# Attention scores in one plain fp32 product instead of two products on split operands

## The reference, cut to what matters

```
q_bucket = sum((q @ proj > 0) * 2**bit)          # k_bucket likewise
mask     = q_bucket[:, None] == k_bucket[None, :]
scores   = where(mask, scale * q @ k.T, -1e9)
attn     = softmax(scores)                       # over the keys
out      = attn @ v                              # fp32
```

## Time and profile before

| | |
|---|---|
| median of 3 runs | 672.47 us (672.25 to 673.8) |
| span of the profiled execution | 672.3 us |
| its mean granted TensorE clock | 0.990 |
| PE busy, of the span | 638.7 us, 95% |
| DVE, ACT, POOL busy | 54%, 46%, 37% |

### The profile page before, as it was taken

How to read it: one execution, slowest core, us unless ns; L and a number is a source line. 1 busy time by engine, 2 the same in 40 slices (tenths; PEclk the granted TensorE clock), 3 DMA queues, 4 the chain that set the end, 5 groups by cost and what they waited for, 6 DMA issues and landing times.

```text
span 672.3 us, 11293 instructions
## 1 busy us (share of the span) xinstructions
PE 638.7 (95%) x3810; PEld 512.0 (76%) x3810; DVE 364.8 (54%) x599; ACT 307.5 (46%) x586; POOL 250.7 (37%) x202
## 2 busy tenths in 40 slices
PE   2899999999999999888999999999999999996998
PEld 1667576766666675888888888889888888885786
DVE  3878786968778785987211111116333333369720
ACT  2877776868686773355322222223222222251132
POOL 6543333334252341844333333326444444342130
PEclk9999999999999999989999999999999999998899
DMA  5822231324132000100222221520222221000102
GB/s 125 248 71 71 71 94 47 94 68 112 56 91 71 0 25 1 48 1 0 64 63 62 62 62 62 188 63 30 65 62 62 62 62 47 1 0 1 62 32 94
DMA packets 34262, 42.08 MB, mean 63 GB/s; under 512 B 3520, under 2 KB 22208, under 8 KB 34240
## 3 DMA queue, kind: packets, MB, share of 16 engines
q1 hardware_dynamic: 32512, 37.77, 19.6%
q0 software_dynamic: 1728, 4.02, 2.3%
HBM read 38.63 MB, written 3.15 MB: 62 GB/s over the span
## 4 chain that ended last, share of the span: by engine, by line
PE 81%; DVE 11%; issue 3%; POOL 2%; ACT 1%; DMA 1%; SPq 0%; DVEq 0%; POOLq 0%; ACTq 0%
PE banks L1457 20%; PE banks L1445 20%; PE banks L1260 10%; PE banks L1243 10%; PE banks L1307 6%; PE banks L1552 5%; DVE row_min L927 2%; PE banks L1199 2%; PE banks L1536 2%; DVE x_then_u_then_gate L1135 2%; PE banks L1380 2%; PE banks L1432 1%; DVE x_then_u_then_gate L1132 1%; DVE probT L342 1%; DVE k_b L920 1%
## 5 line engine op out<-in xcount | busy, mean ns | idle before, releaser
L1122 DVE SCALAR_TENSOR_TENSOR h_lo<-banks,h_hi 128x512 fp32r<-128x512 f32 x64 | 35.5, 558 | 180.8 <-ACT h_hi L825 180.8
L927 DVE TENSOR_REDUCE row_min<-banks 128x1 f32<-128x768 f32 x96 | 91.3, 956 | 44.9 <-PE banks L1243 44.4
L676 ACT ACTIVATE prob<-banks,row_min 128x768 f32<-128x768 f32 x96 | 87.0, 906 | 30.7 <-DVE row_min L927 30.7
L1445 PE MATMUL banks<-unT_hi,w_hi 128*128 128x512 f32 (+1 forms) x256 | 86.3, 337 | 0.0
L1445 PE MATMUL banks<-unT_hi,w_lo 128*128 128x512 f32 (+1 forms) x256 | 86.2, 337 | 0.0
L1445 PE MATMUL banks<-unT_lo,w_hi 128*128 128x512 f32 (+1 forms) x256 | 86.1, 336 | 0.0
L1307 PE MATMUL banks<-ident,prob 128*128 128x128 f32 x576 | 79.7, 274 | 2.5 <-DVE probT L342 1.5
L501 POOL TENSOR_TENSOR k_b<-k_raw,k_a 64x768 fp32r<-64x768 f32 x16 | 29.2, 1826 | 125.6 <-ACT k_a L659 125.6
L1307 PEld LDWEIGHTS banks<-ident,prob 128*128 128x128 f32 x576 | 67.3, 140 | 10.3 <-ACT probT L342 2.6
L563 POOL TENSOR_TENSOR w_lo<-w_stage,w_hi 128x512 fp32r<-128x512 f32 x32 | 43.6, 1363 | 82.9 <-ACT w_hi L741 82.9
L1260 PE MATMUL banks<-probT,v_in 128*64 128x384 f32 x384 | 72.3, 498 | 0.7 <-ACT outT L686 0.7
(11 more groups left out here) (148 smaller groups left out, 1223.5 us busy)
## 6 DMA issues: line engine op xcount, KB each, us to landing
w_stage<-in_moe_w_ch SPq DMA_DIRECT2D x64, 256.0 KB, 2.9
q_raw<-in_q SPq DMA_DIRECT2D x32, 192.0 KB, 3.3
k_raw<-in_k SPq DMA_DIRECT2D x32, 192.0 KB, 3.6
v_in<-in_v SPq DMA_DIRECT2D x16, 192.0 KB, 2.4
out<-y_out SPq DMA_DIRECT2D x12, 256.0 KB, 2.0
seq_tables_sb<-in_dft POOLq DMA_DIRECT2D x6, 386.0 KB, 3.5
wvo_stage<-in_moe_w_val SPq DMA_DIRECT2D x1, 1024.0 KB, 5.2
wvo_stage<-in_moe_w_out SPq DMA_DIRECT2D x1, 1024.0 KB, 7.9
```

Of the source, the lines that this page charges most:

```text
L676: act.activation(prob[s % 2][:, :, :], s_tile(s), ACT.Exp, bias=row_min[:, s:s + 1], scale=-1.0, accum_out=row_sum[:, s:s + 1]).then_inc(e ...
L927: dve.tensor_reduce(row_min[:, s:s + 1], s_tile(s), AX.XY, ALU.min).then_inc(min_ready, 1)
L1122: dve.scalar_tensor_tensor(out=h_lo[:, slot, at:at + size], in0=h_bank[c], scalar=0.0, in1=h_hi[:, slot, at:at + size].bitcast(F32), op0=A ...
L1445: op = pe.matmul(h_bank[c], w_[:, slot, kb, :], x_[:, kb, at:at + size], start=(kb == 0 and m == 0), stop=(kb == KB - 1 and m == 2))
```

## The change

The two products become one product of plain fp32 operands `q_op` and `k_op` of 128 partitions: upper half the scaled q and k themselves, lower half the one-hot rows as before. q and k are loaded once each, into the upper and the lower half of one tile `qk_raw[h]`. The bits are made from that tile without waiting for the scaled q: `w_q` now lies in the upper and `w_k` in the lower half, for which `proj` is loaded twice. POOL only scales q into `q_op` (64 partitions); ACT only copies k from the lower half of the raw tile to the upper half of `k_op`; the roundings, remainders and the copy of q go.

```
-            q_a[h] = sb(f"q_a{h}", [P, S], F32R, region)
-            q_b[h] = sb(f"q_b{h}", [P, S], F32R, region)
-            k_a[h] = sb(f"k_a{h}", [P, S], F32R, region)
-            k_b[h] = sb(f"k_b{h}", [P, S], F32R, region)
+            q_op[h] = sb(f"q_op{h}", [P, S], F32, region)
+            k_op[h] = sb(f"k_op{h}", [P, S], F32, region)
...
-                for dst, src in ((q_raw, q_v), (k_raw, k_v)):
-                    for half in range(2):
-                        sp.dma_start(dst[h][half * D:half * D + D, :], src[2 * i + h]).then_inc(qk_loaded[h], 16)
+                for half, src in enumerate((q_v, k_v)):
+                    sp.dma_start(qk_raw[h][half * D:half * D + D, :], src[2 * i + h]).then_inc(qk_loaded[h], 16)
...
-            sp.dma_start(proj_sb[:, :], proj).then_inc(proj_loaded, 16)
+            for half in range(2):
+                sp.dma_start(proj_sb[half * D:half * D + D, :], proj).then_inc(proj_loaded, 16)
...
             def scale_q(i, h):
-                pool.wait_ge(qk_loaded[h], 64 * (i + 1))
-                need(pool, lo_done, 2 * operands(i, h))
-                pool.tensor_tensor(q_raw[h][:, :], q_raw[h][:, :], minus_scale[:, :].broadcast_to([P, S]),
+                pool.wait_ge(qk_loaded[h], 32 * (i + 1))
+                need(pool, scores_done, (i - 1) * SLOTS + (T * (h + 1)))
+                pool.tensor_tensor(q_op[h][0:D, :], qk_raw[h][0:D, :], minus_scale[0:D, :].broadcast_to([D, S]),
                                    ALU.mult).then_inc(q_scaled, 1)
-            def split_qk(i, h):         # and its calls
...
-            def round_k(i, h):          # and round_q, copy_q, with their calls
+            def copy_k(i, h):
+                need(act, qk_loaded[h], 32 * (i + 1))
                 need(act, scores_done, (i - 1) * SLOTS + (T * (h + 1)))
+                act.copy(k_op[h][0:D, :], qk_raw[h][D:2 * D, :]).then_inc(k_copied, 1)
...
-            dve.tensor_scalar(w_q[top, 0:BITS], proj_sb[:, :], -1.0, None, ALU.mult).then_inc(w_ready, 1)
-            dve.tensor_copy(w_k[top, 0:BITS], proj_sb[:, :]).then_inc(w_ready, 1)
+            dve.tensor_copy(w_q[top, 0:BITS], proj_sb[top, :]).then_inc(w_ready, 1)
+            dve.tensor_copy(w_k[low, 0:BITS], proj_sb[low, :]).then_inc(w_ready, 1)
...
-                    need(pe, q_scaled, operands(i + nxt, h) + 1)
+                    pe.wait_ge(qk_loaded[h], 32 * (i + nxt + 1))
...
-                    need(pe, hi_done, 3 * operands(i, h) + 3)
-                    need(pe, lo_done, 2 * operands(i, h) + 2)
+                    need(pe, k_copied, operands(i, h) + 1)
+                    need(pe, q_scaled, operands(i, h) + 1)
...
-                for lhs, rhs, start in ((q_a[h], k_a[h], True), (q_b[h], k_b[h], False)):
-                    for c in range(2):
-                        op = pe.matmul(s_tile(s)[:, c, :], lhs[:, rows], rhs[:, c * HALF:(c + 1) * HALF],
-                                       start=start, stop=not start)
+                for c in range(2):
+                    op = pe.matmul(s_tile(s)[:, c, :], q_op[h][:, rows], k_op[h][:, c * HALF:(c + 1) * HALF],
+                                   start=True, stop=True)
```

More of the change, by code:

```diff
@@ L101, in attention_fft_ffn_gate_kernel @@
         outT = sb("outT", [P, HALF], F32, region)
-        proj_sb = sb("proj_sb", [D, BITS], F32, region)
+        proj_sb = sb("proj_sb", [P, BITS], F32, region)
         code_ones = sb("bucket_ones_sb", [P, 1], F32, region)
@@ L108, in attention_fft_ffn_gate_kernel @@
         row_inv = sb("row_inv", [P, 2, HT, 2], F32, region)
-        q_a, q_b, k_a, k_b = ([None, None] for _ in range(4))
+        q_op, k_op = [None, None], [None, None]
         for h in (1, 0):
-            q_a[h] = sb(f"q_a{h}", [P, S], F32R, region)
-            q_b[h] = sb(f"q_b{h}", [P, S], F32R, region)
-            k_a[h] = sb(f"k_a{h}", [P, S], F32R, region)
-            k_b[h] = sb(f"k_b{h}", [P, S], F32R, region)
+            q_op[h] = sb(f"q_op{h}", [P, S], F32, region)
+            k_op[h] = sb(f"k_op{h}", [P, S], F32, region)
         bits_sb = sb("bits_sb", [P, HALF], F32R, region)
@@ L122, in attention_fft_ffn_gate_kernel @@
         w_k = sb("w_k", [P, GROUP], F32, region)
-        q_raw = [sb(f"q_raw{h}", [P, S], F32, region) for h in range(2)]
-        k_raw = [sb(f"k_raw{h}", [P, S], F32, region) for h in range(2)]
+        qk_raw = [sb(f"qk_raw{h}", [P, S], F32, region) for h in range(2)]
         region.close()
@@ L179, in attention_fft_ffn_gate_kernel @@
         q_scaled = sem("q_scaled")
-        hi_done = sem("hi_done")
-        lo_done = sem("lo_done")
+        k_copied = sem("k_copied")
         scores_done = sem("scores_done")
@@ L489, in scale_q @@
             def scale_q(i, h):
-                pool.wait_ge(qk_loaded[h], 64 * (i + 1))
-                need(pool, lo_done, 2 * operands(i, h))
-                pool.tensor_tensor(q_raw[h][:, :], q_raw[h][:, :], minus_scale[:, :].broadcast_to([P, S]),
+                pool.wait_ge(qk_loaded[h], 32 * (i + 1))
+                need(pool, scores_done, (i - 1) * SLOTS + (T * (h + 1)))
+                pool.tensor_tensor(q_op[h][0:D, :], qk_raw[h][0:D, :], minus_scale[0:D, :].broadcast_to([D, S]),
                                    ALU.mult).then_inc(q_scaled, 1)
-            def split_qk(i, h):
[L498 to L507, removed]
             pool.wait_ge(consts_ready, 9)
             scale_q(0, 0)
-            split_qk(0, 0)
             scale_q(0, 1)
-            split_qk(0, 1)
-            scale_q(1, 0)
             for dst, src in ((fc_hi, feat_cos_hi), (fc_lo, feat_cos_lo), (fs_hi, feat_sin_hi),
@@ L525, in _ @@
             with pool.Fori(1, NP - 1) as i:
-                split_qk(i, 0)
-                scale_q(i, 1)
+                scale_q(i, 0)
                 pool.dma_start(seq_tab[:, bass.ds(2 * (i - 1), 2), :], seq_tables[:, bass.ds(2 * (i - 1), 2), :])\
                     .then_inc(tables_loaded, 16)
-                split_qk(i, 1)
-                scale_q(i + 1, 0)
-            split_qk(NP - 1, 0)
+                scale_q(i, 1)
+            scale_q(NP - 1, 0)
             scale_q(NP - 1, 1)
-            split_qk(NP - 1, 1)
             def fold_rows(b):
@@ L550, in _ @@
             wait_drained(pool, NP - 1, (3, "O"))
-            pool.wait_ge(lo_done, 4 * NP)
+            pool.wait_ge(q_scaled, 2 * NP)
             pool.wait_ge(fold_edge, 3)
@@ L653, in _ @@
         def _(act):
-            def round_k(i, h):
-                need(act, qk_loaded[h], 64 * (i + 1))
+            def copy_k(i, h):
+                need(act, qk_loaded[h], 32 * (i + 1))
                 need(act, scores_done, (i - 1) * SLOTS + (T * (h + 1)))
[L659 to L668, removed]
+                act.copy(k_op[h][0:D, :], qk_raw[h][D:2 * D, :]).then_inc(k_copied, 1)
             def softmax_exp(i, s):
@@ L695, in round_parts @@
                     act.wait_ge(scores_done, NP * SLOTS)
-                    act.wait_ge(lo_done, 4 * NP)
+                    act.wait_ge(q_scaled, 2 * NP)
                 act.wait_ge(fold_sum, 3 * (b + 1))
@@ L715, in pair @@
                     if s % 6 == 0 and last + nxt < 2:
-                        round_k(i + nxt, h)
+                        copy_k(i + nxt, h)
                     if last < 2:
                         softmax_exp(i, s)
[L719 to L722, removed]
                     if s == 1 and not (isinstance(i, int) and i == 0):
@@ L726, in pair @@
                         copy_outT(i, 1)
-            round_k(0, 0)
-            round_q(0, 0)
-            copy_q(0, 0)
+            copy_k(0, 0)
             pair(0, 0)
@@ L892, in _ @@
             top, low = slice(0, D), slice(D, 2 * D)
-            dve.wait_ge(proj_loaded, 16)
+            dve.wait_ge(proj_loaded, 32)
             dve.wait_ge(consts_ready, 3)
-            dve.tensor_scalar(w_q[top, 0:BITS], proj_sb[:, :], -1.0, None, ALU.mult).then_inc(w_ready, 1)
-            dve.tensor_copy(w_k[top, 0:BITS], proj_sb[:, :]).then_inc(w_ready, 1)
+            dve.tensor_copy(w_q[top, 0:BITS], proj_sb[top, :]).then_inc(w_ready, 1)
+            dve.tensor_copy(w_k[low, 0:BITS], proj_sb[low, :]).then_inc(w_ready, 1)
             dve.wait_ge(ones_loaded, 16)
@@ L918, in prepare @@
                     cols = slice(c * HALF, c * HALF + HALF)
-                    dve.tensor_scalar(q_b[h][low, cols], src[top, :], code_ones[top, :], None, ALU.is_equal)
-                    op = dve.tensor_scalar(k_b[h][low, cols], src[low, :], code_ones[low, :], BIG,
+                    dve.tensor_scalar(q_op[h][low, cols], src[top, :], code_ones[top, :], None, ALU.is_equal)
+                    op = dve.tensor_scalar(k_op[h][low, cols], src[low, :], code_ones[low, :], BIG,
                                            ALU.not_equal, ALU.mult)
@@ L1196, in bits @@
                 for group in range(4):
-                    w, x = ((w_q, q_raw), (w_k, k_raw))[group // 2]
-                    c = group % 2
```

(3 more changed lines are left out.)

## The result

The changed kernel takes 716.6 us (median of 4 runs, 714.8 to 717.0) against 673.1 for the kernel before (672.3 to 674.0) beside it: a ratio of 1.064, interval 1.0615 to 1.066. It is 43 us slower; 723 was forecast, in a range of 713 to 735. Its profiled execution has a span of 715.3 us.

A forecast was written before the change was run, and what follows sets the result against it. PE, busy 95% of the span, was taken as the bound. Six loop pairs +39.6, first pair +6.2, last pair +6.1, start -1.5 give +50.4 on 672.3: 722.7, said as 723 us, range 713 to 735.

The forecast's parts named there:

- the fourth rival: More is won beside the product (emptier ACT and POOL, score overhead shrinking, 8 us): about 714; chance 0.12.
- The passes: Score product on PE: a full-width tile takes 8 passes of 384 columns where it took 4.
- bare loads: Score product: weight loads can't hide under the matmul before, 54 us more, about 775; chance 0.06.
- the free fp32 product: Score product: one record is one pass, so a tile stays at four passes, about 670; chance 0.05.
- The price of a tile: Score tile on PE: from 0.81 to 1.45 us, +0.64, with 0.17 overhead carried over; 61.4 us for 96 tiles.
- L1260's 1.44: Check on the tile: four two-pass steps of 64-column products take 1.44 us, against 0.81 + 0.64 = 1.45.
- What is swallowed: Slots 9 and 10: PE's 1.1 us of waits behind DVE vanish; a pair +6.6, six pairs +39.6.
- Pair 0: First pair: slots 0 to 2 +3.4, slots 3 to 10 +2.2, slot 11 +0.6; +6.2 us in all.
- Pair 7: Last pair: slots 0 to 5 +3.8, slots 6 to 11 +2.3 with some stalls left; +6.1 us.
- The start: Before PE's first bits: proj loads issued earlier and POOL's earlier scaling frees DVE; 1.5 us gained.
- The rest at nothing: Work removed from ACT and POOL, ACT's copy of k, halved loads, stages after attention: no cost of their own.
- the third rival: Slots without v: DVE or the loop of waits stays the bound, so stalls stay, about 733; chance 0.12.

The follow-up runs named there:

- the quarters: The changed kernel with its fp32 score product cut into four column pieces of 192 instead of two of 384: 716.0 us, ratio 1.064.
- The old product twice: The kernel before, with each tile's four fp32r score matmuls issued twice: 725.9 us, ratio 1.078.
- The copy moved in the kernel before: The kernel before, with ACT taking the second copy of the transposed probabilities from DVE in slots 8 and 10 too: 672.3 us, ratio 0.998.
- the work put back: The changed kernel with two copies per head on ACT and two subtractions on POOL added into tiles nobody reads: 717.0 us, ratio 1.065.
- the version with one rounded product: The changed kernel with q_op and k_op of type fp32r instead of plain fp32: 654.2 us, ratio 0.972.

## Why the prediction was right

The direction, the cause and the stated range held. Two of the prediction's own marks did not: 716.6 lies below the forecast's narrow range of 718 to 728, and the prediction was to be wrong if pairs grew by other than 6 to 7.7 us; they grew by 5.8. The time is nearer to the fourth rival (714, part of the 0.17 us of overhead falls away) than to the 723 that I named. So the number of passes was right and the overhead on them was not. Point by point:

- *The passes.* Right: a plain fp32 record is two passes of its columns, 0.32 us for 384, and a full-width tile is eight passes. Of the rivals that hung on it both are out, bare loads by the quarters and the free fp32 product by the tile's own time. (The Trainium skill, "FP8 and Floating Point Precision", TensorE Precision Notes, gives true fp32 four passes; the two records of two passes agree.)
- *The price of a tile.* The term that was too large: +0.64 forecast, +0.58 measured, as the mean of the ten slots of a pair without waits (slot 8 from 1.65 to 2.22, slots with products with v 0.56 to 0.60 more, slot 5 0.67, slots 6 and 7 0.54 and 0.48). I carried the 0.17 us over the four bare passes into the new tile. "The old product twice" splits it: 0.013 for each fp32r record and about 0.1 for the tile. In the new tile nearly nothing is left for each record, and the 0.1 is there in eight slots of twelve. The check by L1260's 1.44 agreed in part by chance, since 0.1 of it stands where 64 and 128 output columns meet. For 96 tiles this is 5 to 6 us too much.
- *What is swallowed.* Right in size: 12 x 0.58 = 7.0, less 1.1, is 5.9, and the pair grew by 5.8. I named DVE as the cause of both waits. The copy moved in the kernel before shows that relief of DVE alone doesn't lift them. That ACT's queue, with the copy of q in it, has a part is read from its timeline; how the 1.1 us divides was not measured.
- *Pair 0* grew by 4.0 (from its first scores to those of pair 1: 14.52 to 40.25 before by the same timeline, 12.83 to 42.53 after), not 6.2. That is the other term too large: slots 0 to 2 grew by 2.2 where I had 3.4. The first two tiles grew by 2.56, as forecast, but the third, for which I had put a price between the two levels, grew by 0.1, and the bits before it got 0.44 shorter, since the clock had risen by then. Slots 3 to 10 swallowed more (+1.2, not +2.2). *Pair 7* grew by 5.5, not 6.1: I had left it stalls in slots 6 to 11, and those now take 12.4 us, which is PE's work alone.
- *The start* won 1.7 us, 1.5 forecast, for the reason given: DVE has `proj` at 5.81 instead of 7.37 and is let go when POOL's scaling ends, at 6.90 instead of 8.72. Not waiting for the scaled q had no part in it.
- *The rest at nothing.* Right, and shown by the work put back. This holds behind the long product. What the removed work is worth with the short one was not tested; there DVE and ACT set the pace, and 4 us came off by moving one copy in two slots.

Sum as measured by the traces: -1.7 + 4.0 + 34.8 (six pairs) + 5.5 = 42.6, against 50.4. All four terms came out below the forecast, by 0.2, 2.2, 4.8 and 0.6, so the range held by its width and not because errors cancelled. One sum of the prediction is slightly off, without effect: the third rival's comes to 732, not 733.

## What to carry to other kernels

Count TensorE's work in passes of columns before counting instructions: two products of a one-pass type cost half of one product of a four-pass type, though they look like twice the work, and the records of the narrower products of the same type in the trace tell the number of passes. Overhead read from records of one type and width doesn't carry over unchanged to others. Work taken from engines that nobody waits for is worth nothing, and an engine at 95% pays each pass in full, but for the waits it already has. If precision allows, the type of an operand is the cheapest edit; once it has made TensorE short, read again which engine the others wait for, since the bound has moved.

## What the runs showed of the hardware

- Eight plain fp32 records of 192 columns, each with a load of 128 rows by 128 columns, ran in 1.30 us, so these loads for all rows were hidden under a running matmul, even at 0.16 us a record.
- Two products of 64 output columns side by side ran at the pace of one of 128 columns: 1.39 against 1.40 us a tile behind other products of 64 columns. Behind and ahead of instructions of 128 columns a tile took 1.44 against 1.30, and the transposes after it 0.81 against 0.65: the surcharge lies at the change of width.
- A tiny DVE operation whose operands lie in SBUF was held until a POOL operation of 1.46 us ended: 1.11 us for 64 x 6 elements and 1.11 us for 128 x 6 where it began 0.4 us after POOL's, 0.65 where it began 0.8 after it (the version with one rounded product), and 0.16 to 0.17 where POOL was idle. Twice it stood on the path.
